# Attention scores by head on two diagonal quarters of the array, in a fused attention and two-layer expert kernel

## What is computed

```python
# q, k, v: (4, 8, 576, 64)
scores = scale * np.matmul(q, k.transpose(0, 1, 3, 2))
rel = pos[:, None] - pos[None, :]
mask = (rel >= 0) & (rel < 64)
scores = np.where(mask, scores, -1000000000.0)
attn = softmax(scores)                      # over the last axis
x = np.matmul(attn, v)                      # reordered to (2304, 512)
h = x @ w_in                                # (512, 2048)
x2 = (h - np.tanh(h)) @ w_out               # (2048, 512)
# logits from unit rows of x2 and expert_emb, argmax picks an expert e
out = gate * (np.maximum(x2 @ w1[e], 0.0) @ w2[e])
```

## Time and profile before

| | |
|---|---|
| median of three runs | 850.33 us |
| the profiled execution's own time | 849.17 us |
| its span, first to last instruction | 847.0 us |
| TensorE (PE) busy | 804.4 us, 95% |
| weight loads (PEld) busy | 694.5 us, 82% |
| VectorE (DVE) busy | 468.0 us, 55% |
| ScalarE (ACT) busy | 368.0 us, 43% |
| GpSimd (POOL) busy | 200.5 us, 24% |

### The profile page before, as it was taken

The page is one execution under the profiler, slowest core; times in us unless marked ns, Lnnn a source line. Parts: engine busy times, 40 slices in busy tenths (PEclk is TensorE's granted clock), DMA queues, the critical chain, the costliest instruction groups (busy, mean ns, idle before and its releaser), DMA issues. The chain is left out here.

```text
span 847.0 us, 16644 instructions
## 1 busy us (share of the span) xinstructions
PE 804.4 (95%) x4680; PEld 694.5 (82%) x4681; DVE 468.0 (55%) x1399; ACT 368.0 (43%) x910; POOL 200.5 (24%) x276
## 2 busy tenths in 40 slices
PE   7899999999999999999999998399999999999992
PEld 6888888888888888888889997278888888888871
DVE  7666645765577567756763665645443251654322
ACT  4554544433443344344442324246444442664333
POOL 4457621223122312131211001301111111111111
PEclk9999999999999999999999999599999999999995
DMA  9972123322332233223206211056271523466110
GB/s 176 238 232 67 40 51 100 76 61 49 99 79 56 50 100 85 52 50 100 69 14 224 75 38 38 27 202 221 73 236 47 185 93 121 152 236 225 49 47 17
DMA packets 106310, 87.87 MB, mean 104 GB/s; under 512 B 79012, under 2 KB 80169, under 8 KB 106242
## 3 DMA queue, kind: packets, MB, share of 16 engines
q1 hardware_dynamic: 98386, 74.92, 30.6%
q0 software_dynamic: 4624, 11.32, 4.4%
q10 hardware_dynamic: 3232, 0.79, 0.5%
HBM read 152.87 MB, written 11.46 MB: 194 GB/s over the span
## 5 line engine op out<-in xcount | busy, mean ns | idle before, releaser
L1259 PE MATMUL banks<-xh,win_h 128*128 128x384 f32 x384 | 135.6, 353 | 0.9 <-issue 0.9
L1260 PE MATMUL banks<-xl,win_h 128*128 128x384 f32 x384 | 129.1, 336 | 0.0
L1261 PE MATMUL banks<-xh,win_l 128*128 128x384 f32 x384 | 129.1, 336 | 0.0
L958 DVE TENSOR_TENSOR gl<-gf,gh 128x384 fp32r<-128x384 f32 x96 | 55.6, 579 | 132.0 <-ACT gh L710 132.0
L1259 PE MATMUL banks<-wout_h,gh 128*128 128x512 f32 x288 | 117.5, 408 | 0.0
L1260 PE MATMUL banks<-wout_l,gh 128*128 128x512 f32 x288 | 114.0, 396 | 0.0
L1261 PE MATMUL banks<-wout_h,gl 128*128 128x512 f32 x288 | 113.5, 394 | 0.0
L703 ACT ACTIVATE gf<-banks 128x384 f32<-128x384 f32 x96 | 47.2, 492 | 152.4 <-PE banks L1261 151.9
L521 POOL TENSOR_TENSOR sm<-sm,rr 128x384 f32<-128x384 f32 x48 | 47.6, 991 | 270.0 <-DVE rr L883 270.0
L710 ACT CAST gh<-gf 128x384 fp32r<-128x384 f32 x96 | 49.2, 512 | 130.4 <-PE banks L1261 112.9
L1136 DVE TENSOR_TENSOR hTl<-banks,hTh 128x512 fp32r<-128x512 f32 x50 | 32.3, 687 | 92.0 <-ACT hTh L807 91.9
(11 more groups left out here) (192 smaller groups left out, 1504.1 us busy)
## 6 DMA issues: line engine op xcount, KB each, us to landing
w1raw<-in_moe_w_dram SPq DMA_DIRECT2D x104, 512.0 KB
w2raw<-in_moe_w_dram SPq DMA_DIRECT2D x104, 512.0 KB
x2T<-unit_embeddings SPq DMA_DIRECT2D x20, 256.0 KB, 3.6
junk<-unit_embeddings SPq DMA_DIRECT2D x20, 256.0 KB, 3.6
x_rows<-x SPq DMA_DIRECT2D x6, 768.0 KB, 5.2
wout_raw<-in_moe_w_out_dram SPq DMA_DIRECT2D x4, 1024.0 KB, 6.8
win_raw<-in_moe_w_in_dram SPq DMA_DIRECT2D x3, 1024.0 KB, 9.8
vw<-in_v_dram SPq DMA_DIRECT2D x16, 192.0 KB, 3.2
```

Source lines behind the costliest of these rows:

```text
L958: dve.tensor_tensor(gl[c % 2][:], gf[c % 2][:], gh[c % 2][:], ALU.subtract).then_inc(g_split, 1)
L1259: pe.matmul(to, sh, mh, start=start, stop=False)
L1260: pe.matmul(to, sh, ml, start=False, stop=False)
L1261: return pe.matmul(to, sl, mh, start=False, stop=stop)
```

## The change

The stationary operand of the scores is taken by head. `qT` holds q for both heads without zero blocks, 64 columns for each window. It is written by one instruction of 128 partitions in place of two of 64, and it needs no zeroing. Each of the three score products becomes two, one for each head: 64 rows by 64 columns of stationary operand, 128 moving columns from the same 64 partitions of `kT`, and an output in the same 64 partitions of PSUM. So head 0 uses the quarter of the array at rows and columns 0 to 63, and head 1 the one at 64 to 127.

```diff
-        qbd = [sb(f"qbd{i}", [P, GB, 2, WINDOW], scope=attn) for i in range(2)]
+        qT = [sb(f"qT{i}", [P, GB, WINDOW], scope=attn) for i in range(2)]
...
             for keys in kT:
-                dve.memset(keys[:, 0, :], 0.0)
-            for i in range(2):
-                dve.memset(qbd[i][:], 0.0).then_inc(pads_zeroed, 1)
+                last = dve.memset(keys[:, 0, :], 0.0)
+            last.then_inc(pads_zeroed, 2)
             dve.wait_ge(pads_zeroed, 2)
...
                 wait(dve, scored, g - 1)
-                for h in range(2):
-                    rows = slice(h * D, (h + 1) * D)
-                    dve.tensor_scalar(qbd[i][rows, :, h, :], psT(g)[rows, :, 0:WINDOW], float(D) ** -0.5, None, ALU.mult)
+                dve.tensor_scalar(qT[i][:], psT(g)[:, :, 0:WINDOW], float(D) ** -0.5, None, ALU.mult)
...
                 for u in range(GB):
-                    last = pe.matmul(psS(g)[:, u, :], qbd[i][:, u, :, :].rearrange("p h c -> p (h c)"), kT[hp][:, u:u + 2, :],
-                                     start=True, stop=True)
+                    for h in range(2):
+                        own = slice(h * D, (h + 1) * D)
+                        last = pe.matmul(psS(g)[own, u, :], qT[i][own, u, :], kT[hp][own, u:u + 2, :], start=True, stop=True)
                 last.then_inc(scored, 1)
```

## The result

The changed kernel takes 862.82 us (median of four runs, 861.61 to 863.37), the kernel before 850.0 us (849.24 to 850.99). The ratio is 1.0146 with a 95% interval from 1.0131 to 1.0160: slower, by 12.8 us where 13.65 were foretold, and 1.1 us under the forecast of 863.9. The profiled execution took 862.63 us, with a span of 860.3.

The account below looks back on a forecast made before the run. TensorE was taken to bound the kernel, with VectorE counting only in the first 42 us. Borders 14.6, start -0.5 and wait -0.45 sum to 13.65 us over 850.33, giving 863.9 us, range 857 to 869.

Parts of the forecast that it names:

- The bound: Whole kernel: TensorE is busy 804.4 of 847.0 us and sets the time; VectorE counts only in the first 42 us.
- The stream: Each score's twelve quarter records run two at a time, six slots of 0.111 us, 0.67 us as before: zero change.
- the serial rival: In 40 scores the heads' quarters run one by one, six more slots each: +27 us, about 891 us; chance 0.08.
- the third one: Rival: more than two score records run at once, three slots instead of six: -13.4 us, 850.5 us; chance 0.10.
- The borders: Entering and leaving the partial shape at 40 scores costs 0.37 us behind transposes, 0.35 between products: 14.6 us more.
- The free rival: Changing shape costs the score nothing, so only the gains at the start remain: 847.7 us; chance 0.12.
- The first 8 groups: Start of the kernel: -2 us from VectorE, +1.0 for shape changes, +0.5 lost to ScalarE: -0.5 us.
- VectorE's part: First 8 groups: one q copy instead of two saves 0.35 us a group, about -2 us by the first attend.
- +1.0: First 8 groups: three steps led by TensorE each pay some 0.33 us for shape changes around the score.
- +0.5: First 8 groups: the part of the gain in us taken as lost to ScalarE, which TensorE already waited for.
- The wait behind them: First dense-layer score: its wait for k's copy shrinks 0.35 us and hides 0.1 us of entry: -0.45 us.
- The sum: Whole kernel: 14.6 - 0.5 - 0.45 = 13.65 us more, giving 863.9 us.

Follow-up runs that it names:

- the experiment with heads outside: The changed kernel with three products of head 0, then three of head 1, in each score: 873.09 us, 10.3 us more than the changed kernel.
- halves: Against the kernel before, each score is six products of 128 rows by 64 columns; block-diagonal operand and both copies stay: 862.58 us, ratio 1.0159.
- the first pair: First profiles of the kernel before and the changed kernel, each profiled once more later; dense layers took 486.9 and 499.8 us.
- the experiment with one copy: The kernel before with q copied by one instruction into one block, scores still three full products: 846.03 us, ratio 0.9970.

## Why the prediction was right, point by point

- **The bound.** TensorE is the whole of the middle, before and after. VectorE's relief of 48 x 0.35 us was worth 2.5 us by itself, and by the profile all of it came in the first 42 us.
- **The stream.** Foretold: two records at a time, six slots of 0.111 us, a term of zero. It is so, and the experiment with heads outside shows that the pairs are the two heads. Two quarters wrote one bank at once, each in its own partitions, at full pace. That puts the serial rival out, and the third one, of three slots. The serial rival had named the Trainium skill, page "TensorEngine Tiling (Array Packing)", section "Restrictions and Gotchas", by which different row tiles cannot access the same PSUM bank at the same time. These rows differ from it, and the measurement decides: two quarters on different rows began within 0.01 us of each other (205.638 and 205.645), and both write the bank of `psS(g)`, where their outputs share no partition.
- **The borders.** This was the deciding term: 14.6 us foretold for 40 scores, 14.3 of it for the 39 without a wait, and 12.8 measured for these. The parts were 0.12 + 0.05 + 0.20 us behind transposes and came out as 0.09 + 0.045 + 0.19. The entry was the mis-sized one. I read it from rows of attend in the first groups, where 0.23 us stood between the last transpose and attend; the score's is 0.20. The whole price is 0.33 us for quarters and for halves behind transposes, 0.33 between products and 0.35 for attend, and one small quarter product costs 0.42 with its own work. So it depends little on how much of the array is used or how much is streamed.
- **The free rival** is out by the same rows. Its argument was that attend's 64 moving columns are too short to cover their loads; scores of 128 moving columns pay nearly the same.
- **The first 8 groups.** -0.5 us foretold. By the profiles the first dense product came 0.9 us earlier in the first pair and 1.4 in the second; by its time the kernel with quarters in these groups alone gained 0.6, with 0.2 more to 1.4 less inside its interval. The two terms behind the -0.5 are less well shown. VectorE's part was 2.3 us in one profile, and of 2.5 by time 0.5 belong to the wait behind. That leaves 1.4 us between 2.0 and 0.6 for the borders, near the +1.0 and +0.5 of the prediction, but the intervals are as wide as that. One profile speaks against it: with halves, which have the borders and both copies, the first dense product came at 34.86, no later than before.
- **The wait behind them.** The -0.45 of the prediction and the 0.47 that was measured agree by luck. Foretold were 0.35 for the copy and 0.10 for an entry hidden in the wait. The copy alone brought 0.47, as the experiment with one copy shows. With its borders that score was to be 0.10 us shorter and was 0.33 shorter. A score that has waited had its first load in the open before the change already (its six records last 0.94 us and not 0.83), so the borders charged it less.
- **The sum** was 13.65 us. By medians it is 12.8, and 13.3 by the spans of the first pair of profiles. These divide, but for rounding, into 12.9 in the dense layers where 14.15 were foretold (the borders less the wait), -0.9 at the start where -0.5 were, and 1.4 behind attention that no step of the prediction had and whose cause is open. The mechanism is as foretold and its main term was too high by a tenth. The total came closer than its parts, since their errors have different signs, and that is luck.

## What to carry to other kernels

Before giving TensorE a smaller shape, look at what stands before and behind it. Going from the full array to a part and back costs a fixed 0.33 us here, against which only streamed columns saved can be set: attend's halves save as much as they cost, the scores' quarters saved none, since six slots of 0.11 us is what the product with zero blocks took as well. If partial shapes are needed, put those of one shape side by side; this rests on one place in one kernel, where the step between them cost nothing, and no kernel here was built that way throughout. And relief on an engine counts only in the stretches where it leads, which a table by stretches shows at once.

## What the runs showed that I had not expected

- With three products of one head ahead of three of the other, TensorE began the second head's records 0.27 us after the first head's, while the third of six was running. It works ahead of program order, but here only by that much, so alternating the heads is still worth 0.27 us a group. Why it began no earlier is not shown.
- A single partial product of 32 moving columns among full ones costs 0.42 us, its own work included.
- Copying two heads in one VectorE instruction of 128 partitions takes 352 ns, exactly what each instruction of 64 partitions took the earlier trace rows.
